# A convolution by Fourier steps with a token-wise network: one PSUM bank for the filter network's products, three PSUM buffers for the fold

## The chip, the cores and the metric

The kernel runs on one core of a Trainium2 chip. The metric is the device time of one execution in microseconds, from its first to its last instruction and what lies around them. Lower is better.

## The reference

`x` and `v` are (2, 12480, 128) in fp32. The first part multiplies them, convolves the product along the sequence with a learned filter, and multiplies by `x` again. The filter comes from a small two-layer network on position embeddings, and fades out along the sequence. The second part is a token-wise network with a rational activation.

```python
h_filt = (np.maximum(pos_emb @ w1, 0.0) @ w2) * np.exp(-0.01 * pos)[:, None]
u = x * v
Uf, Hf = np.fft.rfft(u, n=2 * S, axis=1), np.fft.rfft(h_filt, n=2 * S, axis=0)
y = np.fft.irfft(Uf * Hf[None, :, :], n=2 * S, axis=1)[:, :S, :]
out = moe(x * y)          # w_in (128, 2048), rational function, w_out (2048, 128)
```

## The kernel before

The transform is split in two steps, N = 192 x 120, so that it becomes matrix products. The kernel has three stages with a barrier between them: the first goes from `x`, `v` and the position embeddings to `bent` in DRAM, the second from `bent` to `back`, the third from `back` through the network to the output. Only the first stage is touched, and what follows is about it alone.

The sequence is seen as 104 rows of J = 120. A block is JB = 4 of these 120 columns, so there are 30 blocks. For a block, the engines do this:

- SP loads `x_s`, `v_s` and `pos_s` (`load`, lines 170 to 177) and stores the result in two halves (`store`, 179 to 186).
- The filter network: PE transposes the embeddings (`transposes`, L305) into `posT_p`; ACT copies them to `posT` (L223); PE multiplies by `w1` (`hidden`, L314) into `hid_p`; ACT applies the ReLU (L230); PE multiplies by `w2` (`filter_rows`, L321) into `filt_p`; DVE multiplies by the window (`filt`, L270), into the filter's columns of `uh`.
- DVE multiplies x and v (`product`, L264) into the other columns of `uh`.
- ACT rounds `uh` to `uh_hi` in two halves (`split_hi`, L239), and POOL subtracts to get `uh_lo` (`split_lo`, L211).
- For each of the four columns, PE folds (`fold_j`, L333): six matmuls of 384 columns into one buffer of `g_p` (two PSUM banks). ACT scales it by a cosine (`cos_part`, L246), DVE adds the sine part in two instructions (`turn`, L283 and L285) to `bent_s`. The second of these frees the buffer: `turned[j % 2]`.

PSUM holds eight banks. `posT_p`, `hid_p` and `filt_p` take one each, `g_p` has two buffers of two banks.

The order on each engine is written out by hand. `pipelined` (lines 86 to 102) runs a list of parts per step; a part with lead n works on the block n ahead. Step b on PE is: `transposes` of block b+2, fold 0 of b, `hidden` of b+2, fold 1 of b, `filter_rows` of b+2, fold 2 of b, fold 3 of b. On ACT: `posT` copy of b+2, cosine part 0 of b, `split_hi(0)` of b+1, ReLU of b+2, cosine part 1, `split_hi(1)` of b+1, cosine parts 2 and 3. On DVE: turn 0, `product` of b+2, turn 1, `filt` of b+2, turns 2 and 3. On SP: the store of b, then the load of b+5, which waits until the product of b+3 has been made. Each engine works through its list in that order; the semaphores between them carry counts of blocks or of folds. In the steady part a hardware loop covers two blocks per pass.

These waits matter for the change: `fold_j` waits for `turned[j % 2]` (L330), that is for the turn two folds before. `transposes` waits until the earlier copy has been taken out of `posT_p` (L302). `hidden` waits in addition for the earlier ReLU (L312), and `filter_rows` for the earlier `filt` (L319).

Of the kernel before, what the change touches and what calls it, by code (L numbers as in the profile page):

```python
# [38 lines left out]
JB = 4  # L39
# [5 lines left out]
SLOTS = 2  # L45
EPS = 1e-6
# [3 lines left out]
assert ROWS * J == SEQ and J_BLOCKS % SLOTS == 0 and K_BLOCKS % SLOTS == 0  # L50
# [22 lines left out]
def hyena_mlp(nc, x, v, pos_emb, w1, w2, w_in, w_out, a, b, tab, out):  # L73
# [30 lines left out]
    with ExitStack() as whole:  # L104
# [22 lines left out]
        with ExitStack() as ctx:  # L127
# [32 lines left out]
            g_done, part_done, turned = sem("g_done"), sem("part_done"), sems("turned")  # L160
# [3 lines left out]
            ITERS = J_BLOCKS // SLOTS  # L164
# [3 lines left out]
            @block.sync  # L168
            def _(sp):
                def load(i, s):  # L170
                    blk = i * SLOTS + s
# [7 lines left out]
                def store(i, s):  # L179
                    blk = i * SLOTS + s  # L180
# [10 lines left out]
                pipelined(sp, ITERS, SLOTS, [(0, store), (LEAD_LOAD, load)])  # L191
                for dst, src in ((spread_s, tab["spread"]), (turn_j, tab["turn_j"]), (unfold_s, tab["unfold"]), (w_in_s, w_in),
                                 (w_out_s, w_out.rearrange("(t p) d -> p t d", p=128)),
                                 (coef, a.rearrange("(o n) -> o n", o=1).to_broadcast([128, 4])),
                                 (den_raw, b.rearrange("(o n) -> o n", o=1).to_broadcast([128, 2]))):
                    sp.dma_start(dst[:], src).then_inc(later_in, 16)
                for out_sem in bent_out:
                    sp.wait_ge(out_sem, 16 * ITERS)

            @block.gpsimd  # L200
            def _(pool):

                for s in range(SLOTS):
                    nc.gpsimd.memset(uh[64:ROWS, s, :, BD:COLS], 0.0).then_inc(pad_zero, 1)

                def split_lo(i, s):
                    for half in range(2):

                        pool.wait_ge(uh_hi_done, (i * SLOTS + s) * 2 + half + 1)
# [4 lines left out]
                pipelined(pool, ITERS, SLOTS, [(0, split_lo)])  # L214

            @block.scalar
            def _(act):
                def posT_copy(i, s):
                    blk = i * SLOTS + s
# [3 lines left out]
                    nc.scalar.activation(posT[:], posT_p[:, 0:JB * FILTER_ROWS], ACT.Copy).then_inc(posT_sb, 1)  # L223

                def relu(i, s):
                    blk = i * SLOTS + s
# [3 lines left out]
                    nc.scalar.activation(hid[:], hid_p[:, 0:JB * FILTER_ROWS], ACT.Relu).then_inc(hid_sb, 1)  # L230

                def split_hi(half):
                    def part(i, s):
                        blk = i * SLOTS + s
# [7 lines left out]
                def cos_part(j):  # L242
                    def part(i, s):
                        n = (i * SLOTS + s) * JB + j
                        act.wait_ge(g_done, n + 1)
                        nc.scalar.activation(part_s[:, j % 2], g_p[0:K1, j % 2, :, 0:COLS], ACT.Copy,  # L246
# [6 lines left out]
                pipelined(act, ITERS, SLOTS, [(LEAD_MAKE, posT_copy), (0, cos_part(0)), (LEAD_SPLIT, split_hi(0)),  # L253
# [4 lines left out]
            def _(dve):  # L258
                def product(i, s):
                    blk = i * SLOTS + s  # L260
                    dve.wait_ge(xv_in[s], 32 * (i + 1))
# [5 lines left out]
                def filt(i, s):  # L267
                    blk = i * SLOTS + s
                    dve.wait_ge(filt_ps, blk + 1)
                    nc.vector.tensor_tensor(  # L270
                        uh[0:FILTER_ROWS, s, :, BD:COLS], filt_p[0:FILTER_ROWS],
# [3 lines left out]
                def turn(j):  # L275
                    def part(i, s):
                        n = (i * SLOTS + s) * JB + j
                        dve.wait_ge(part_done, n + 1)
                        if j % 2 == 0:
                            dve.wait_ge(bent_out[s * 2 + j // 2], 16 * i)  # L280
                        sin = turn_k[:, bass.ds(n, 1), 1:2].rearrange("p a b -> p (a b)")
                        neg = turn_k[:, bass.ds(n, 1), 2:3].rearrange("p a b -> p (a b)")
                        nc.vector.scalar_tensor_tensor(out=bent_s[:, s, j, 0, :], in0=g_p[0:K1, j % 2, 1, 0:COLS], scalar=sin,  # L283
                                                       in1=part_s[:, j % 2, 0, :], op0=ALU.mult, op1=ALU.add)
                        nc.vector.scalar_tensor_tensor(out=bent_s[:, s, j, 1, :], in0=g_p[0:K1, j % 2, 0, 0:COLS], scalar=neg,  # L285
                                                       in1=part_s[:, j % 2, 1, :], op0=ALU.mult, op1=ALU.add
                                                       ).then_inc(turned[j % 2], 1)
# [6 lines left out]
                pipelined(dve, ITERS, SLOTS, [(0, turn(0)), (LEAD_MAKE, product), (0, turn(1)), (LEAD_MAKE, filt),  # L294
# [3 lines left out]
            def _(pe):  # L298
                def transposes(i, s):
                    pe.wait_ge(pos_in[s], 16 * (i + 1))  # L300
                    if positive(i * SLOTS + s):
                        pe.wait_ge(posT_sb, i * SLOTS + s)  # L302
                    pe.sem_inc(pe_passed, 1)
                    for j in range(JB):
                        mm = nc.tensor.transpose(posT_p[:, j * FILTER_ROWS:(j + 1) * FILTER_ROWS], pos_s[:, s, j, :],  # L305
# [3 lines left out]
                def hidden(i, s):  # L309
# [4 lines left out]
                    nc.tensor.matmul(hid_p[:, 0:JB * FILTER_ROWS], w1_s[:], posT[:], start=True, stop=True).then_inc(hid_ps, 1)  # L314

                def filter_rows(i, s):
                    pe.wait_ge(hid_sb, i * SLOTS + s + 1)
                    if positive(i * SLOTS + s):
                        pe.wait_ge(filt_done, i * SLOTS + s)  # L319
                    for j in range(JB):  # L320
                        mm = nc.tensor.matmul(filt_p[0:FILTER_ROWS, j, :], hid[:, j * FILTER_ROWS:(j + 1) * FILTER_ROWS],  # L321
# [3 lines left out]
                def fold_j(j):  # L325
                    def part(i, s):
                        blk = i * SLOTS + s
                        if j % 2 == 0:
                            pe.wait_ge(uh_lo_done, blk * 2 + j // 2 + 1)
                        pe.wait_ge(turned[j % 2], blk * (JB // 2) + j // 2)  # L330
                        for c in range(2):
                            for n, (w, f) in enumerate(((fold_lo, uh_hi), (fold_hi, uh_hi), (fold_hi, uh_lo))):
                                mm = nc.tensor.matmul(g_p[0:K1, j % 2, c, 0:COLS], w[:, c * K1:(c + 1) * K1], f[:, s, j, :],  # L333
                                                      start=(n == 0), stop=(n == 2))
# [5 lines left out]
                pipelined(pe, ITERS, SLOTS, [(LEAD_MAKE, transposes), (0, fold_j(0)), (LEAD_MAKE, hidden), (0, fold_j(1)),  # L340
# [615 lines left out]
```

## Time and profile before

| what | value |
|---|---|
| median of three runs | 2239.24 us (2235.86 to 2241.52) |
| profiled execution | 2240.67 us |
| its span, first to last instruction | 2238.9 us |
| busy in the span: PE, DVE, ACT, POOL | 92%, 81%, 81%, 85% |
| first stage, by the timeline | to about 276 us |
| second stage | to about 640 us |
| third stage | the rest |

The busy shares are means over three stages that have little in common, so they say little about one of them. Times in the rows further down are microseconds from the start of the span. In a timeline row the first number is the start, the second the length, and the bracket tells how long the engine had been idle and what ended that; a row can merge several instructions of one kind ("x4"). A matmul's length includes its way through the array, so the next one starts before it ends.

### The profile page before, as it was taken

The numbers are of one execution on the slowest core, as the hardware profiler recorded it, in microseconds if no ns is written. First come the engines' busy times: TensorE is split into PE (matmuls) and PEld (weight loads), VectorE is DVE, ScalarE is ACT, GpSimd is POOL, SyncE is SP. The second block draws the span as 40 slices with busy tenths as digits, with TensorE's granted clock in tenths as the row PEclk, the third lists the DMA queues.
The fourth block names the chain that finished last, engine by engine and source line by source line (L and its number), as shares of the span: only waits on it lengthen the run. The fifth ranks groups of instructions, "written<-read, shape, count | busy, mean of one in ns | idle before, by whom it ended". The sixth has DMA issues, their size and how long they took to land. (4 is left out here: it accounts for less than half of the span.)

```text
span 2238.9 us, 33664 instructions
## 1 busy us (share of the span) xinstructions
PE 2048.9 (92%) x8964; PEld 1458.6 (65%) x8964; DVE 1805.7 (81%) x2271; ACT 1822.0 (81%) x2431; POOL 1894.0 (85%) x1218
## 2 busy tenths in 40 slices
PE   7888769999968999999999999999999999999997
PEld 5666559999955666666666666666666666666664
DVE  4777648888847888888888888888888888888887
ACT  4767646666638999999999999999999999899997
POOL 3666558888838999999999999999999999999997
PEclk9999979999979999999999999999999999999999
DMA  6888677666640111111111111111111111111100
GB/s 164 260 258 259 209 163 176 176 176 176 176 108 11 30 34 30 29 35 49 29 29 29 29 29 29 29 31 31 29 31 46 37 29 29 29 29 29 29 8 16
DMA packets 65724, 175.02 MB, mean 78 GB/s; under 512 B 5046, under 2 KB 8414, under 8 KB 62686
## 3 DMA queue, kind: packets, MB, share of 16 engines
q1 hardware_dynamic: 65694, 174.67, 29.4%
q8 instruction: 13, 0.21, 0.0%
q14 instruction: 17, 0.14, 0.0%
HBM read 102.89 MB, written 71.76 MB: 78 GB/s over the span
## 5 line engine op out<-in xcount | busy, mean ns | idle before, releaser
L625 POOL TENSOR_TENSOR den<-slope,mag 128x832 f32<-128x832 f32 x480 | 946.2, 1971 | 43.5 <-POOL slope L617 6.9
L878 PE MATMUL acc_p<-g_s,w_out_k 128*128 128x416 f32 x1920 | 784.1, 531 | 88.3 <-DVE g_s L785 83.5
L752 DVE SCALAR_TENSOR_TENSOR num<-square,level,h_p 128x832 f32<-128x832 f32 x480 | 517.8, 1079 | 90.1 <-ACT square L659 79.3
L617 POOL TENSOR_SCALAR slope<-mag,den_c 128x832 f32<-128x832 f32 x480 | 500.3, 1042 | 98.9 <-ACT mag L650 70.2
L785 DVE SCALAR_TENSOR_TENSOR g_s<-num,ratio,r_p 128x832 f32<-128x832 f32 x480 | 516.0, 1075 | 83.2 <-ACT r_p L676 54.6
L878 PEld LDWEIGHTS acc_p<-g_s,w_out_k 128*128 128x128 f32 x1920 | 332.6, 189 | 373.4 <-issue 221.8
L659 ACT ACTIVATE square<-h_p,centre 128x832 f32<-128x832 f32 x480 | 459.0, 956 | 128.7 <-DVE mag L747 112.5
L867 PE MATMUL h_p<-xy_hi,w_lo 128*128 128x416 f32 x960 | 459.1, 478 | 5.6 <-DVE num L752 4.3
L669 ACT ACTIVATE den<-den 128x832 f32<-128x832 f32 x480 | 431.1, 898 | 0.0
L676 ACT ACTIVATE r_p<-den 128x832 f32<-128x832 f32 x480 | 417.4, 870 | 12.9 <-DVE g_s L785 12.9
L867 PE MATMUL h_p<-xy_lo,w_hi 128*128 128x416 f32 x960 | 338.0, 352 | 0.0
L867 PE MATMUL h_p<-xy_hi,w_hi 128*128 128x416 f32 x960 | 337.5, 352 | 0.0
L867 PEld LDWEIGHTS h_p<-xy_hi,w_lo 128*128 128x128 f32 x960 | 181.6, 189 | 143.1 <-DVE num L752 113.0
L211 POOL TENSOR_TENSOR uh_lo<-uh,uh_hi 104x768 fp32r<-104x768 f32 x60 | 151.6, 2544 | 113.9 <-ACT uh_hi L239 113.8
L747 DVE TENSOR_SCALAR mag<-h_p 128x832 int32<-128x832 int32 x240 | 244.1, 1017 | 0.0
L409 POOL TENSOR_TENSOR bin_lo<-bin_s,bin_hi 120x768 fp32r<-120x768 f32 x96 | 178.3, 1858 | 71.2 <-ACT bin_hi L428 71.2
L867 PEld LDWEIGHTS h_p<-xy_hi,w_hi 128*128 128x128 f32 x960 | 182.4, 190 | 52.2 <-issue 51.4
L650 ACT ACTIVATE mag<-h_p 128x832 f32<-128x832 f32 x240 | 205.8, 857 | 3.2 <-PE h_p L867 3.2
L867 PEld LDWEIGHTS h_p<-xy_lo,w_hi 128*128 128x128 f32 x960 | 181.4, 189 | 1.4
L246 ACT ACTIVATE part_s<-g_p,turn_k 96x768 f32<-96x768 f32 x120 | 107.7, 898 | 83.0 <-PE g_p L333 83.0
L498 PE MATMUL x_p<-bin_hi,spread_lo 120*120 120x384 f32 x384 | 130.2, 339 | 28.5 <-POOL bin_lo L409 28.5
L498 PE MATMUL x_p<-bin_lo,spread_hi 120*120 120x384 f32 x384 | 130.6, 340 | 0.0
(79 smaller groups left out, 2805.4 us busy)
## 6 DMA issues: line engine op xcount, KB each, us to landing
bent<-bent_s SPq DMA_DIRECT2D x60, 576.0 KB, 4.8
bin_s<-bent SPq DMA_DIRECT2D x24, 1440.0 KB, 9.7
x_s<-in_x SPq DMA_DIRECT2D x60, 416.0 KB
back<-back_s SPq DMA_DIRECT2D x24, 960.0 KB, 7.8
vin_s<-back SPq DMA_DIRECT2D x30, 768.0 KB, 5.8
v_s<-in_v SPq DMA_DIRECT2D x30, 416.0 KB
out<-o_s SPq DMA_DIRECT2D x60, 208.0 KB
pos_s<-in_pos_emb SPq DMA_DIRECT2D x30, 88.0 KB
```

The costliest lines, as they stand in the source:

```text
L498: mm = nc.tensor.matmul(to, w, f, start=(n == 0), stop=(n == len(every) - 1))
L617: nc.gpsimd.tensor_scalar(slope[:, q % DEEP], mag[:, q % DEEP], den_c[:, 1:2], den_c[:, 0:1], ALU.mult, ALU.add).then_inc(slope_done, 1)
L625: nc.gpsimd.tensor_tensor(den[:, q % DEEP], slope[:, q % DEEP], mag[:, q % DEEP], ALU.mult).then_inc(den_done, 1)
L650: nc.scalar.activation(mag[:, q % DEEP], h_p[:, q % 2, :, 0:TOK], ACT.Abs).then_inc(mag_act, 1)
L659: nc.scalar.activation(square[:, q % SQUARES], h_p[:, q % 2, :, 0:TOK], ACT.Square, bias=centre[:]).then_inc(square_done, 1)
L669: nc.scalar.activation(den[:, q % DEEP], den[:, q % DEEP], ACT.Ln, bias=1.0 + EPS).then_inc(log_done, 1)
L676: nc.scalar.activation(r_p[:, :, 0:TOK], den[:, q % DEEP], ACT.Exp, scale=-1.0).then_inc(r_done, 1)
L747: nc.vector.tensor_scalar(mag[:, q % DEEP].bitcast(I32), h_p[:, q % 2, :, 0:TOK].bitcast(I32), NO_SIGN, None, ALU.bitwise_and).then_inc(ma ...
L752: nc.vector.scalar_tensor_tensor(out=num[:, q % NUMS], in0=square[:, q % SQUARES], scalar=level[:], in1=h_p[:, q % 2, :, 0:TOK], op0=ALU.a ...
L785: nc.vector.scalar_tensor_tensor(out=g_s[:, q % DEEP], in0=num[:, q % NUMS], scalar=ratio[:, 0:1], in1=r_p[:, :, 0:TOK], op0=ALU.add, op1= ...
L867: mm = nc.tensor.matmul(h_p[:, q % 2, t, 0:TOK], w[:, at:at + 128], f[:, s, b_, :], start=(n == 0), stop=(n == 2))
L878: mm = nc.tensor.matmul(acc_p[:, 0:TOK], w_out_k[:, ft], g_s[:, q % DEEP, t], start=(ft == 0), stop=(ft == FT - 1))
```

## The change

The three products of the filter network go to one bank, `mlp_p`, one after another. Two banks come free, and `g_p` gets a third buffer. Folds are numbered through, and fold n uses buffer n mod 3, so the loop is written over 6 blocks (24 folds) instead of 2; every count and slot is rewritten for that. The leads and the order of parts on each engine stay the same.

```diff
+RING = 3
...
-            part_s = sb("part_s", [K1, 2, 2, COLS])
+            part_s = sb("part_s", [K1, RING, 2, COLS])
...
-            posT_p = ps("posT_p", [ORDER, 512])
-            hid_p = ps("hid_p", [ORDER, 512])
-            filt_p = ps("filt_p", [128, JB, D])
-            g_p = ps("g_p", [128, 2, 2, 512])
+            mlp_p = ps("mlp_p", [128, 512])
+            g_p = ps("g_p", [128, RING, 2, 512])
...
-            ITERS = J_BLOCKS // SLOTS
+            PER = SLOTS * RING
+            ITERS = J_BLOCKS // PER
...
                     for half in range(2):
-                        sp.wait_ge(turned[1], blk * (JB // 2) + half + 1)
+                        last = q * JB + (half + 1) * (JB // 2) - 1
+                        sp.wait_ge(turned[last % RING], i * (PER * JB // RING) + last // RING + 1)
...
-                        nc.scalar.activation(part_s[:, j % 2], g_p[0:K1, j % 2, :, 0:COLS], ACT.Copy,
+                        r = (q * JB + j) % RING
+                        nc.scalar.activation(part_s[:, r], g_p[0:K1, r, :, 0:COLS], ACT.Copy,
...
-                                                       ).then_inc(turned[j % 2], 1)
+                                                       ).then_inc(turned[r], 1)
...
-                def transposes(i, s):
-                    pe.wait_ge(pos_in[s], 16 * (i + 1))
-                    if positive(i * SLOTS + s):
-                        pe.wait_ge(posT_sb, i * SLOTS + s)
+                def transposes(i, q):
+                    s = q % SLOTS
+                    pe.wait_ge(pos_in[s], 16 * (i * RING + q // SLOTS + 1))
+                    if positive(i * PER + q):
+                        pe.wait_ge(filt_done, i * PER + q)
...
-                    pe.wait_ge(posT_sb, i * SLOTS + s + 1)
-                    if positive(i * SLOTS + s):
-                        pe.wait_ge(hid_sb, i * SLOTS + s)
+                    pe.wait_ge(posT_sb, i * PER + q + 1)
...
-                    pe.wait_ge(hid_sb, i * SLOTS + s + 1)
-                    if positive(i * SLOTS + s):
-                        pe.wait_ge(filt_done, i * SLOTS + s)
+                    pe.wait_ge(hid_sb, i * PER + q + 1)
...
-                        pe.wait_ge(turned[j % 2], blk * (JB // 2) + j // 2)
+                        r = (q * JB + j) % RING
+                        pe.wait_ge(turned[r], i * (PER * JB // RING) + (q * JB + j) // RING)
```

## Rows read from the trace of the kernel before

**Rows 1.** Windows, warm stretch; busy us by engine, granted clock, DMA share, GB/s.
```profile
46.79:235.92 189.13, 163.64 (x874) 115.08 (x875) 142.59 (x230) 132.16 (x186) 118.52 (x46) 1.00 0.83 254
```

**Rows 2.** Waits from 40 to 230 us: waiter, releaser, total us, times, longest.
```profile
POOL uh_lo L211 <- ACT uh_hi L239: 77.6, 24, 7.0
...
PE g_p L333 <- DVE bent_s L285: 10.2, 23, 0.7
PE g_p L333 <- POOL uh_lo L211: 8.8, 11, 0.8
```

**Rows 3.** Timeline of one period: start us, length us, engine, line, idle before.
```profile
235.92 0.38 PE L333 MATMUL g_p<-uh_hi,fold_lo 104*96 104x384 f32 x1 [0.72 <-DVE bent_s L285]
...
237.32 0.90 ACT L246 ACTIVATE part_s<-g_p,turn_k 96x768 f32<-96x768 f32 x1 [1.04 <-PE g_p L333]
...
238.12 0.83 ACT L239 ACTIVATE uh_hi<-uh 104x768 fp32r<-104x768 f32 x1
...
238.38 0.61 DVE L283 SCALAR_TENSOR_TENSOR bent_s<-g_p,turn_k,part_s 96x384 f32<-96x384 f32 x1 [1.15 <-ACT part_s L246]
...
238.85 0.45 ACT L230 ACTIVATE hid<-hid_p 64x352 f32<-64x352 f32 x1
...
239.35 1.10 PE L321 MATMUL filt_p<-w_s,hid 64*88 64x128 f32 x8 [0.21 <-ACT hid L230]
239.43 1.21 DVE L264 TENSOR_TENSOR uh<-x_s,v_s 104x1024 f32<-104x1024 f32 x1
...
240.38 0.42 PE L333 MATMUL g_p<-uh_hi,fold_lo 104*96 104x384 f32 x1
...
240.57 0.61 DVE L283 SCALAR_TENSOR_TENSOR bent_s<-g_p,turn_k,part_s 96x384 f32<-96x384 f32 x1
...
241.62 0.68 DVE L270 TENSOR_TENSOR uh<-filt_p,window 88x512 f32<-88x512 f32 x1
...
241.75 0.41 PE L333 MATMUL g_p<-uh_hi,fold_lo 104*96 104x384 f32 x1
241.81 0.90 ACT L246 ACTIVATE part_s<-g_p,turn_k 96x768 f32<-96x768 f32 x1 [0.90 <-PE g_p L333]
...
242.87 0.47 PE L305 MATMUL posT_p<-ident,pos_s 88*64 88x88 f32 x4
242.87 0.61 DVE L283 SCALAR_TENSOR_TENSOR bent_s<-g_p,turn_k,part_s 96x384 f32<-96x384 f32 x1 [0.57 <-ACT part_s L246]
243.17 0.90 ACT L246 ACTIVATE part_s<-g_p,turn_k 96x768 f32<-96x768 f32 x1 [0.46 <-PE g_p L333]
...
243.97 0.44 ACT L223 ACTIVATE posT<-posT_p 64x352 f32<-64x352 f32 x1
...
244.16 0.38 PE L333 MATMUL g_p<-uh_hi,fold_lo 104*96 104x384 f32 x1 [0.82 <-POOL uh_lo L211]
```

**Rows 4.** Timeline, blocks 1 and 2: transposes and first folds on PE.
```profile
33.71 0.79 PE L305 MATMUL posT_p<-ident,pos_s 88*64 88x88 f32 x4
...
34.48 0.60 PE L333 MATMUL g_p<-uh_hi,fold_lo 104*96 104x384 f32 x1
...
46.79 0.39 PE L333 MATMUL g_p<-uh_hi,fold_lo 104*96 104x384 f32 x1 [0.36 <-DVE bent_s L285]
```

**Rows 5.** Timeline, start of the stage: second transposes and first filter product.
```profile
16.32 0.80 PE L305 MATMUL posT_p<-ident,pos_s 88*64 88x88 f32 x4
16.43 0.69 DVE L270 TENSOR_TENSOR uh<-filt_p,window 88x512 f32<-88x512 f32 x1 [4.83 <-PE filt_p L321]
```

**Rows 6.** Timeline, end of the stage: folds 0 of blocks 28, 29; last turn.
```profile
260.61 0.38 PE L333 MATMUL g_p<-uh_hi,fold_lo 104*96 104x384 f32 x1 [1.12 <-POOL uh_lo L211]
...
267.63 0.38 PE L333 MATMUL g_p<-uh_hi,fold_lo 104*96 104x384 f32 x1 [0.80 <-DVE bent_s L285]
...
275.22 0.60 DVE L285 SCALAR_TENSOR_TENSOR bent_s<-g_p,turn_k,part_s 96x384 f32<-96x384 f32 x1
```

**Rows 7.** Windows, stretch behind the stage, columns as in rows 1.
```profile
278.00:305.30 27.30, 4.07 (x13) 4.07 (x14) 2.73 (x2) 3.88 (x4) 3.58 (x2) 0.50 0.89 208
```

More of the change, by code:

```diff
@@ L48 @@
 NO_SIGN = 0x7FFFFFFF
-assert ROWS * J == SEQ and J_BLOCKS % SLOTS == 0 and K_BLOCKS % SLOTS == 0
+assert ROWS * J == SEQ and J_BLOCKS % (SLOTS * RING) == 0 and K_BLOCKS % SLOTS == 0
 assert N >= SEQ + FILTER_ROWS * J - 1 and FILTER_ROWS <= ROWS <= 128 and TOK <= 512
@@ L169, in _, with load @@
             def _(sp):
-                def load(i, s):
-                    blk = i * SLOTS + s
+                def load(i, q):
+                    blk, s = i * PER + q, q % SLOTS
                     if positive(blk - 1):
@@ L190, in _ @@
                     sp.dma_start(dst[:], src).then_inc(consts_in, 16)
-                pipelined(sp, ITERS, SLOTS, [(0, store), (LEAD_LOAD, load)])
+                pipelined(sp, ITERS, PER, [(0, store), (LEAD_LOAD, load)])
                 for dst, src in ((spread_s, tab["spread"]), (turn_j, tab["turn_j"]), (unfold_s, tab["unfold"]), (w_in_s, w_in),
@@ L197, in _ @@
                 for out_sem in bent_out:
[L198 removed]
+                    sp.wait_ge(out_sem, 16 * (J_BLOCKS // SLOTS))
             @block.gpsimd
@@ L204, in _, with split_lo @@
                     nc.gpsimd.memset(uh[64:ROWS, s, :, BD:COLS], 0.0).then_inc(pad_zero, 1)
-                def split_lo(i, s):
+                def split_lo(i, q):
+                    s = q % SLOTS
                     for half in range(2):
-                        pool.wait_ge(uh_hi_done, (i * SLOTS + s) * 2 + half + 1)
+                        pool.wait_ge(uh_hi_done, (i * PER + q) * 2 + half + 1)
                         at = slice(half * (JB // 2), (half + 1) * (JB // 2))
@@ L212, in split_lo, with posT_copy @@
                                                 ALU.subtract).then_inc(uh_lo_done, 1)
-                pipelined(pool, ITERS, SLOTS, [(0, split_lo)])
+                pipelined(pool, ITERS, PER, [(0, split_lo)])
             @block.scalar
             def _(act):
-                def posT_copy(i, s):
-                    blk = i * SLOTS + s
+                def posT_copy(i, q):
+                    s = q % SLOTS
+                    blk = i * PER + q
                     act.wait_ge(posT_ps, blk + 1)
@@ L222, in posT_copy, with relu @@
                         act.wait_ge(hid_ps, blk)
-                    nc.scalar.activation(posT[:], posT_p[:, 0:JB * FILTER_ROWS], ACT.Copy).then_inc(posT_sb, 1)
-                def relu(i, s):
-                    blk = i * SLOTS + s
+                    nc.scalar.activation(posT[:], mlp_p[0:ORDER, 0:JB * FILTER_ROWS], ACT.Copy).then_inc(posT_sb, 1)
+                def relu(i, q):
+                    s = q % SLOTS
+                    blk = i * PER + q
                     act.wait_ge(hid_ps, blk + 1)
@@ L229, in relu, with part @@
                         act.wait_ge(filt_ps, blk)
-                    nc.scalar.activation(hid[:], hid_p[:, 0:JB * FILTER_ROWS], ACT.Relu).then_inc(hid_sb, 1)
+                    nc.scalar.activation(hid[:], mlp_p[0:ORDER, 0:JB * FILTER_ROWS], ACT.Relu).then_inc(hid_sb, 1)
                 def split_hi(half):
-                    def part(i, s):
-                        blk = i * SLOTS + s
+                    def part(i, q):
+                        s = q % SLOTS
+                        blk = i * PER + q
                         act.wait_ge(filt_done, blk + 1)
@@ L252, in _ @@
                 nc.scalar.activation(fold_hi[:], fold[:], ACT.Copy).then_inc(split_done, 1)
-                pipelined(act, ITERS, SLOTS, [(LEAD_MAKE, posT_copy), (0, cos_part(0)), (LEAD_SPLIT, split_hi(0)),
+                pipelined(act, ITERS, PER, [(LEAD_MAKE, posT_copy), (0, cos_part(0)), (LEAD_SPLIT, split_hi(0)),
                                               (LEAD_MAKE, relu), (0, cos_part(1)), (LEAD_SPLIT, split_hi(1)),
@@ L258, in _, with product @@
             def _(dve):
-                def product(i, s):
-                    blk = i * SLOTS + s
-                    dve.wait_ge(xv_in[s], 32 * (i + 1))
+                def product(i, q):
+                    s = q % SLOTS
+                    blk = i * PER + q
+                    dve.wait_ge(xv_in[s], 32 * (i * RING + q // SLOTS + 1))
                     if positive(blk - 1):
@@ L293, in _ @@
                 nc.vector.tensor_tensor(fold_lo[:], fold[:], fold_hi[:].bitcast(F32), ALU.subtract).then_inc(split_done, 1)
-                pipelined(dve, ITERS, SLOTS, [(0, turn(0)), (LEAD_MAKE, product), (0, turn(1)), (LEAD_MAKE, filt),
+                pipelined(dve, ITERS, PER, [(0, turn(0)), (LEAD_MAKE, product), (0, turn(1)), (LEAD_MAKE, filt),
                                               (0, turn(2)), (0, turn(3))])
@@ L298, in _, with hidden, filter_rows @@
             def _(pe):
-                def transposes(i, s):
-                    pe.wait_ge(pos_in[s], 16 * (i + 1))
-                    if positive(i * SLOTS + s):
-                        pe.wait_ge(posT_sb, i * SLOTS + s)
+                def transposes(i, q):
+                    s = q % SLOTS
+                    pe.wait_ge(pos_in[s], 16 * (i * RING + q // SLOTS + 1))
+                    if positive(i * PER + q):
+                        pe.wait_ge(filt_done, i * PER + q)
                     pe.sem_inc(pe_passed, 1)
                     for j in range(JB):
-                        mm = nc.tensor.transpose(posT_p[:, j * FILTER_ROWS:(j + 1) * FILTER_ROWS], pos_s[:, s, j, :],
+                        mm = nc.tensor.transpose(mlp_p[0:ORDER, j * FILTER_ROWS:(j + 1) * FILTER_ROWS], pos_s[:, s, j, :],
                                                  ident[0:FILTER_ROWS, 0:FILTER_ROWS])
                     mm.then_inc(posT_ps, 1)
-                def hidden(i, s):
-                    pe.wait_ge(posT_sb, i * SLOTS + s + 1)
-                    if positive(i * SLOTS + s):
-                        pe.wait_ge(hid_sb, i * SLOTS + s)
+                def hidden(i, q):
+                    s = q % SLOTS
+                    pe.wait_ge(posT_sb, i * PER + q + 1)
                     pe.sem_inc(pe_passed, 1)
-                    nc.tensor.matmul(hid_p[:, 0:JB * FILTER_ROWS], w1_s[:], posT[:], start=True, stop=True).then_inc(hid_ps, 1)
-                def filter_rows(i, s):
-                    pe.wait_ge(hid_sb, i * SLOTS + s + 1)
-                    if positive(i * SLOTS + s):
-                        pe.wait_ge(filt_done, i * SLOTS + s)
+                    nc.tensor.matmul(mlp_p[0:ORDER, 0:JB * FILTER_ROWS], w1_s[:], posT[:], start=True, stop=True).then_inc(hid_ps, 1)
+                def filter_rows(i, q):
+                    s = q % SLOTS
+                    pe.wait_ge(hid_sb, i * PER + q + 1)
                     for j in range(JB):
-                        mm = nc.tensor.matmul(filt_p[0:FILTER_ROWS, j, :], hid[:, j * FILTER_ROWS:(j + 1) * FILTER_ROWS],
+                        mm = nc.tensor.matmul(mlp_p[0:FILTER_ROWS, j * D:(j + 1) * D], hid[:, j * FILTER_ROWS:(j + 1) * FILTER_ROWS],
                                               w2_s[:], start=True, stop=True)
@@ L325, in fold_j, with part @@
                 def fold_j(j):
-                    def part(i, s):
-                        blk = i * SLOTS + s
+                    def part(i, q):
+                        s = q % SLOTS
+                        blk = i * PER + q
                         if j % 2 == 0:
                             pe.wait_ge(uh_lo_done, blk * 2 + j // 2 + 1)
-                        pe.wait_ge(turned[j % 2], blk * (JB // 2) + j // 2)
+                        r = (q * JB + j) % RING
+                        pe.wait_ge(turned[r], i * (PER * JB // RING) + (q * JB + j) // RING)
                         for c in range(2):
-                            for n, (w, f) in enumerate(((fold_lo, uh_hi), (fold_hi, uh_hi), (fold_hi, uh_lo))):
-                                mm = nc.tensor.matmul(g_p[0:K1, j % 2, c, 0:COLS], w[:, c * K1:(c + 1) * K1], f[:, s, j, :],
-                                                      start=(n == 0), stop=(n == 2))
+                            for term, (w, f) in enumerate(((fold_lo, uh_hi), (fold_hi, uh_hi), (fold_hi, uh_lo))):
+                                mm = nc.tensor.matmul(g_p[0:K1, r, c, 0:COLS], w[:, c * K1:(c + 1) * K1], f[:, s, j, :],
+                                                      start=(term == 0), stop=(term == 2))
                         mm.then_inc(g_done, 1)
@@ L339, in _ @@
                 pe.wait_ge(split_done, 2)
-                pipelined(pe, ITERS, SLOTS, [(LEAD_MAKE, transposes), (0, fold_j(0)), (LEAD_MAKE, hidden), (0, fold_j(1)),
+                pipelined(pe, ITERS, PER, [(LEAD_MAKE, transposes), (0, fold_j(0)), (LEAD_MAKE, hidden), (0, fold_j(1)),
                                              (LEAD_MAKE, filter_rows), (0, fold_j(2)), (0, fold_j(3))])
```

33 lines of the change are left out of this document (18 added, 15 removed).

## The prediction

> **What bounds the kernel now.** The change lies in the first stage alone, so I read the stage by itself: its windows first, then who waits for whom in it, then one period instruction by instruction. From the fold of block 2 on, no engine is full: in 189 us PE is busy 164 (its busy time counts the pipelined tail of each matmul), DVE 143, ACT 132, POOL 119, and the DMA engines are at 0.83 [rows 1]. What is to be seen: everything is partly idle, so a chain that closes on itself sets the period, and no engine's work does. The waits say where PE stands: it waits for DVE's turn (L285), and in nearly as many microseconds for POOL's `uh_lo` [rows 2]. The second I take to be wrongly named: the first half of `uh_lo`, which `fold_j(0)` needs, is ready long before, and only the end of the second half falls beside the end of the turn. POOL itself stands idle for 77.6 us waiting for ACT, so it isn't what is late.
>
> The period is read from fold 0 at 235.92 to the next fold 0 at 244.16, 8.24 us [rows 3]. Follow back what each start waited for. Fold 0 waits for turn 2 of the block before, because there are two PSUM buffers; turn 2 for the cosine part 2; that for fold 2; fold 2 stands on PE behind `filter_rows`; that waits for the ReLU; the ReLU stands on ACT behind `split_hi(0)`, that behind cosine part 0, and that waits for fold 0. In steps, from the starts in [rows 3]: fold 0 to cos 0 1.40, to split 0.80, to ReLU 0.73, to filter_rows 0.50, to fold 2 1.03, to cos 2 1.43, to turn 2 1.06, to the next fold 0 1.29. Sum 8.24: the whole period is explained. Fold 0 of block 2 starts at 46.79 and of block 28 at 260.61 [rows 4, 6], 26 periods of 8.22.
>
> Before 46 us the same chain does not bind. Fold 0 of blocks 1 and 2 start at 34.48 and 46.79, 12.31 apart, and the same matmul takes 0.60 there and 0.39 afterwards [rows 4]: the array is at the lower of its two levels, 1.2 GHz, and PE's own queue fills the period. (The clock column has no entry for the time before its first change; the matmul's length tells.)
>
> **The change, part by part.**
>
> Third PSUM buffer, removed wait: fold n waits for turn n-3 instead of n-2. Fold 0 of the next block then needs turn 1 of this one. Taking fold 0 as time 0, turn 1 starts at 4.65 [rows 3], so with the 1.29 of above it frees the buffer at 5.94. The last three links (1.43 + 1.06 + 1.29 = 3.78) leave the chain.
>
> What is late next: PE's own order. Fold 2 starts 4.46 after fold 0, as before, since cos 0, split, ReLU and filter_rows are not touched. Behind it come fold 3, the transposes for two blocks ahead, and the next fold 0. A fold takes PE 1.12 until the next thing can start (fold 3 to transposes, 241.75 to 242.87 [rows 3]). Fold 3 now needs only turn 0, which starts at 2.46 and frees its buffer before 3.75: no wait. So fold 3 at 5.58, transposes at 6.70. From transposes to fold 0 without a wait the warm trace has nothing; at the low clock it is 0.77 (33.71 to 34.48 [rows 4]). Half of that, 0.39, is the lower bound, all of it the upper; I take 0.50, near the lower, because four small matmuls scale with the clock and only the issue gap doesn't. New period 4.46 + 1.12 + 1.12 + 0.50 = **7.20**, against 8.22: 1.02 saved per block.
>
> One bank for three products, added wait: the transposes now wait for `filt_done` of the block before; until now they waited only for the copy out of their own bank (`posT_sb`). Queued behind them on PE is fold 0, and behind it everything. `filt` starts at 5.70 and takes 0.68 [rows 3], so with 0.1 for the semaphore the wait ends at 6.48, and PE reaches it at 6.70: 0.22 of slack, cost nothing. What hides it is fold 3. If that cover goes, each tenth costs 26 x 0.1 = 2.6 us. The waits dropped in `hidden` and `filter_rows` were met already: nothing.
>
> The start of the stage has no such cover. The second transposes start at 16.32, while the first `filt` starts at 16.43 and takes 0.69 [rows 5]: they would wait until 17.2, 0.9 later. The third transposes stand the same way to the second `filt`, and fold 0 of block 0 stands behind them. Cost 2 x 0.9 = 1.8 us; bounds 0 (if the first operands are late anyway) and 2.5. Against this the 0.36 that fold 0 of block 2 waits for DVE goes [rows 4].
>
> The loop over 6 blocks instead of 2, the shared semaphores counted by thirds, and SP's `store` waiting for the third's own semaphore: SP waits for the same turns as before, 1 and 3. No DMA is added or moved on SP's or POOL's queue. Cost 0; bounds: a loop jump saved or a longer body fetched, less than 1 us either way from how exactly 26 periods agree with the sum of one.
>
> Other queues at 7.20: ACT would start cos 3 at 5.58 + 1.42 = 7.00 and copy `posT` at 7.80 (0.80 after it, as at 243.17 and 243.97 [rows 3]), done at 8.24, before cos 0 of the next block is due at 8.60. DVE would begin the next turn 0 at 9.66 and is done with turn 3 by 9.3. DMA: 0.83 x 8.22 = 6.8 us of transfers per block, 0.95 of a period of 7.20. Loads are issued five blocks ahead, so a queue that is nearly full delays nothing yet.
>
> End of the stage: fold 0 of blocks 28 and 29 start 7.02 apart and the last turn starts 7.59 after the second [rows 6]. With three buffers and no filter work the chain for block 28 is fold 0, cos 0 and split (2.20), cos 1 (0.73 more), turn 1 (1.06), release (1.29): 5.2, saving 1.8. In block 29 fold 3 waits for turn 0 (2.46 + 1.29 = 3.75) where it now waits for turn 1; to the last turn 3.8 + 1.42 + 1.06 + 0.53 = 6.8, saving 0.8. The last full period has no transposes behind it, 0.5 more.
>
> **Sum:** 26 x 1.02 = 26.5; + 0.5 + 1.8 + 0.8 = 29.6; - 1.8 at the start, + 0.36: **28.2 us**. The stages behind begin after a barrier and are not changed; they shift as a whole. The profiled execution took 2240.67 and would take 2212.5; it lies 1.4 above the median of the three runs, so from the median 2239.24 - 28.2 = **2211.0**.
>
> **Rivals.**
>
> A, *DMA becomes the bound.* For: 0.95 of the period needed. Against: the same engines reach 0.89 over a 27 us stretch with other work [rows 7], and the transfers of a block are queued in time. If 0.90 is the most they give here, the period is 6.82/0.90 = 7.58, the gain 26 x 0.64 + 1.3 = 18, the time 2221. Chance 0.14.
>
> B, *the new wait takes the old one's place*, or the third buffer is never used. DVE must bring `filt` before 6.70; if `filt` came 1.24 later than in [rows 3], the period would be what it was and the time within 6 us of 2239. For: only 0.22 of slack, and product and turn 1 stand ahead of `filt` on DVE. Against: its chain from fold 0 (1.40 + 1.06 + 1.05 + 1.14 + 1.05 to `filt`) has no step that the change makes longer. Chance 0.08. The Trainium skill (TensorE: Matmul & The Clock Gate, HAM oscillation) tells of a matmul kernel where more PSUM buffering gave no further gain. By that the sum would be 0; here the trace speaks against it, since PE's named wait in this stage is for exactly that buffer [rows 2].
>
> C, *slower: the array falls to 1.2 GHz inside the stage.* PE now waits on one bank between copy and product, and cycles through three buffers. A block at the low clock costs 12.31 instead of 7.20 [rows 4], 5.1 more. From 6 such blocks on (28.2/5.1) the gain is gone; with half of the 26 low it is 2211 + 13 x 5.1 = 2277. The trace shows such a fall when PE had stopped at the end of the stage: the clock is 0.50 from 278.0 to 305.3 with PE busy for 4.07 [rows 7]. Against: with waits in every block the clock stays 1.00 through 189 us [rows 1], and the change makes PE denser. Chance 0.07. The Trainium skill speaks for C (the same page, A second HAM failure mode: psum-queue depth-cycling): cycling through PSUM banks leaves small idle gaps between groups of matmuls, and the clock then swings. By that rule the kernel before should swing as well, and rows 1 show that it doesn't.
>
> D, *the clock rises earlier.* Blocks 0 and 1 run at 12.3. If the rise falls ahead of them both, 2 x 5.1 = 10 us more are saved: 2201. Chance 0.05. A rise later by 3 us costs about 1.
>
> **The numbers.** Forecast 0.66, A 0.14, B 0.08, C 0.07, D 0.05. The forecast's own bounds: transposes to fold 0 between 0.39 and 0.77 gives 26 x (-0.11 to +0.27) = -2.9 to +7; runs lie 5.7 apart (2235.86 to 2241.52), so 3 either way. That makes 2205 to 2220; with A and part of D **2202 to 2224**. About 0.3% (6.7 us) is what a measurement can tell from no change. Faster 0.85 (forecast, A, D), same 0.08 (B), slower 0.07 (C).
>
> **What would show it.** In the profile after: fold 0 to fold 0 about 7.2; PE's wait for L285 nearly gone and no wait for `filt` (L270) past the first blocks; fold 3 right behind fold 2; DMA share about 0.95 in the same stretch; fold 0 of block 0 later by 1.8; clock 1.00 from about 46 us to the stage's end. Wrong if the period is above 7.6 (then see whether DVE waits for a load, or PE for `filt`), or if the clock shows 0.50 inside the stage.

## The result and the profile after

The changed kernel takes 2198.32 us in the median of 4 runs (2197.26 to 2199.37), against 2237.78 for the kernel before (4 runs, 2235.86 to 2241.52). The ratio is 0.982, with a 95% interval of 0.9806 to 0.9834: 39.5 us less, where 28.2 were forecast. The direction was right; the size was 11 us short and the time lies below the forecast range. In later comparisons, with more runs of the kernel before, its median was 2240.3 to 2241.5, so the gain is rather 41 to 43 us. In the two profiled executions the spans are 2238.9 and 2195.5, 43.4 apart.

The window of the warm stretch of the kernel after, as [rows 1] (columns: stretch, its length, busy us of PE, weight loads, DVE, ACT and POOL, granted clock, DMA share, GB/s):

```profile
44.22:216.14 171.92, 167.76 (x951) 125.88 (x950) 152.91 (x251) 143.89 (x201) 129.09 (x51) 1.00 0.93 308
```

PE is now busy for 168 of 172 us, and the DMA engines for 0.93 instead of 0.83. In the waits of that stretch (40 to 200 us), both lines of [rows 2] in which PE waits at the fold, for DVE's turn and by name for POOL, are absent, and so is any wait of PE for `filt`:

```profile
POOL uh_lo L213 <- ACT uh_hi L244: 45.2, 24, 6.0
ACT part_s L253 <- PE g_p L345: 20.6, 47, 0.9
DVE bent_s L294 <- ACT part_s L253: 17.7, 45, 0.6
...
PEld mlp_p L331 <- ACT hid L234: 8.5, 24, 0.6
PE mlp_p L325 <- ACT posT L226: 3.9, 23, 0.2
```

One period on the timeline, the counterpart of [rows 3] (L345 is the fold, L253 the cosine part, L244 the rounding, L234 the ReLU, L331 `filter_rows`, L325 `hidden`, L317 the transposes, L226 the copy of `posT`, L279 `filt`):

```profile
188.09 0.40 PE L345 MATMUL g_p<-uh_hi,fold_lo 104*96 104x384 f32 x1
...
188.94 0.44 ACT L226 ACTIVATE posT<-mlp_p 64x352 f32<-64x352 f32 x1
...
189.49 0.90 ACT L253 ACTIVATE part_s<-g_p,turn_k 96x768 f32<-96x768 f32 x1
...
189.53 0.77 PE L325 MATMUL mlp_p<-posT,w_s 64*64 64x352 f32 x2 [0.17 <-ACT posT L226]
...
190.23 0.42 PE L345 MATMUL g_p<-uh_hi,fold_lo 104*96 104x384 f32 x1
190.29 0.83 ACT L244 ACTIVATE uh_hi<-uh 104x768 fp32r<-104x768 f32 x1
...
191.03 0.45 ACT L234 ACTIVATE hid<-mlp_p 64x352 f32<-64x352 f32 x1
...
191.52 1.10 PE L331 MATMUL mlp_p<-w_s,hid 64*88 64x128 f32 x8
...
192.56 0.41 PE L345 MATMUL g_p<-uh_hi,fold_lo 104*96 104x384 f32 x1
...
193.68 0.33 PE L345 MATMUL g_p<-uh_hi,fold_lo 104*96 104x384 f32 x1
...
193.80 0.68 DVE L279 TENSOR_TENSOR uh<-mlp_p,window 88x512 f32<-88x512 f32 x1
...
193.98 1.94 ACT L253 ACTIVATE part_s<-g_p,turn_k 96x768 f32<-96x768 f32 x2 [0.69 <-PE g_p L345]
...
194.72 0.47 PE L317 MATMUL mlp_p<-ident,pos_s 88*64 88x88 f32 x4
...
194.97 0.40 PE L345 MATMUL g_p<-uh_hi,fold_lo 104*96 104x384 f32 x1
```

Fold 0 to fold 0 is 188.09 to 194.97, **6.88 us** (8.24 before, 7.20 forecast). The start of the stage, as [rows 4] and [rows 5]:

```profile
22.88 0.69 DVE L279 TENSOR_TENSOR uh<-mlp_p,window 88x512 f32<-88x512 f32 x1 [4.37 <-PE mlp_p L331]
...
23.71 0.77 PE L317 MATMUL mlp_p<-ident,pos_s 88*64 88x88 f32 x4 [0.87 <-DVE uh L279]
...
35.76 0.79 PE L317 MATMUL mlp_p<-ident,pos_s 88*64 88x88 f32 x4
...
36.26 0.61 PE L345 MATMUL g_p<-uh_hi,fold_lo 104*96 104x384 f32 x1
...
43.12 0.47 PE L317 MATMUL mlp_p<-ident,pos_s 88*64 88x88 f32 x4
...
43.38 0.40 PE L345 MATMUL g_p<-uh_hi,fold_lo 104*96 104x384 f32 x1
```

The transposes of step 0 (23.71) wait for `filt`, by name. Fold 0 of block 1 starts at 36.26, where it was 34.48: 1.78 later. In parts: the first transposes start 0.26 later (11.29 against 11.03, both waiting for the first load), from there to fold 0 of block 0 it takes 1.79 more (12.91 against 11.12), which is the wait for `filt`, and block 0 takes 0.27 less (12.06 against 12.33). But fold 0 of block 2 starts at 43.38, where it was 46.79: block 1 took 7.12 instead of 12.31. The first matmul of fold 0 is 0.61 long in block 1 and 0.40 in block 2, so the array's rise from 1.2 to 2.4 GHz lies between them; the clock record of this execution has it at 36.8 us, that of the kernel before at 45.9. (All rises below are the first change in the clock record, on the scale of the timeline; the expectations call this one 36.5.) And the end of the stage, as [rows 6]: fold 0 of block 28, and the last instruction of the last turn.

```profile
221.93 0.34 PE L345 MATMUL g_p<-uh_hi,fold_lo 104*96 104x384 f32 x1
...
233.29 0.60 DVE L296 SCALAR_TENSOR_TENSOR bent_s<-g_p,turn_k,part_s 96x384 f32<-96x384 f32 x1
```

**Where the 43.4 us came from**, and what had been forecast for each:

| part | before | after | gain | forecast |
|---|---|---|---|---|
| to fold 0 of block 1 | 34.48 | 36.26 | -1.8 | -1.8 |
| to fold 0 of block 2 | 12.31 | 7.12 | +5.2 | +0.4 |
| 26 periods, to fold 0 of block 28 | 213.8 | 178.6 | +35.3 | +27.0 |
| to the last turn | 14.6 | 11.4 | +3.3 | +2.6 |
| everything behind | 1963.7 | 1962.2 | +1.5 | 0 |

The last line is no gain. Over the profiles of all kernels here it lies between 1961.8 and 1965.7, without order. So two terms were off: the period by 8.3 us, and the block in which the clock rises by 4.8.

### The profile page after: what moved, and what is told of

Same layout as the page of the kernel before. It is cut to its first block and busy times, and to the rows that moved or that the text cites. A ratio compares the mean times of both kernels' runs of the same rounds, so it can differ in the third digit from the quotient of the medians.

```text
span 2195.5 us, 33367 instructions
## 1 busy us (share of the span) xinstructions
PE 2032.1 (93%) x8964; PEld 1456.4 (66%) x8964; DVE 1803.5 (82%) x2271; ACT 1822.5 (83%) x2431; POOL 1894.3 (86%) x1218
## 5 line engine op out<-in xcount | busy, mean ns | idle before, releaser
L253 ACT ACTIVATE part_s<-g_p,turn_k 96x768 f32<-96x768 f32 x120 | 107.7, 898 | 38.6 <-PE g_p L345 31.9
L858 PE MATMUL m_p<-vin_s,unfold 96*104 96x512 f32 x240 | 116.6, 609 | 15.1 <-DMA vin_s<-back 13.9
```

## The experiments

Two theories stood at the outset. The first: the third buffer makes all of the gain, the shared bank costs 2 us at the start, and the chain of the forecast is right but for the sizes. Its rival: something else has a part, the longer loop body, POOL's `uh_lo`, the transfers, or the clock. Periods below are means between the copies of `posT` for blocks 5 and 27 (22 periods, in one profile of each kernel); by that measure the kernel before has 8.222 and the changed one 6.883.

**E1, shared bank with two buffers, loop over 6.** `GB` is 2; the slots of `part_s` and the counts of `turned` go by `GB` too (not shown).

```diff
-            g_p = ps("g_p", [128, RING, 2, 512])
+            g_p = ps("g_p", [128, GB, 2, 512])
```

> The changed kernel with two fold buffers instead of three: the shared bank and the loop over 6 blocks stay. Theory (all of the gain is the third buffer's, the shared bank costs only at the start): period 8.2 us as before, start later by about 2, total within 3 us of the kernel before, 2236 to 2241. Rival (the longer loop body or the shared bank brings part of the gain): period under 8.0, total under 2232. If the earlier rise of the clock (36.5 instead of 45.9 us) comes from the third buffer, it stays late here.

Measured: 2238.85 (10 runs, 2236.03 to 2245.21), ratio 0.9994 [0.9979, 1.0008]. Period 8.143. The third buffer is what matters: without it there is no gain. The clock rose at 35.6 us in this profile, so an early rise doesn't need the third buffer. The period is 0.08 shorter than before, which asked for E4.

**E2, filter rows in a bank of their own, three buffers.** The transposed embeddings and the hidden layer still share one, and the total is eight banks. The second edit below is in `transposes`; `filter_rows` waits for `filt_done` again (not shown).

```diff
+            filt_p = ps("filt_p", [128, 512])
...
-                        pe.wait_ge(filt_done, i * PER + q)
+                        pe.wait_ge(hid_sb, i * PER + q)
```

> The changed kernel, but only the transposed embeddings and the hidden layer share a bank; the filter rows get a bank of their own, and the fold keeps three buffers. The transposes wait for the ReLU before them instead of for the window product. Theory: period 6.89 as in the changed kernel, the start of the stage earlier by 1.8, total 2196.5. Rival (the wait for the window product costs in every block too): period under 6.8, total under 2193.

Measured: 2197.36 (2195.75 to 2199.18), beside 2199.30 for the changed kernel in the same comparison (2196.62 to 2201.44). Period 6.895. The copy of `posT` in step 0 starts at 22.27 instead of 24.55, 2.28 earlier. But 0.50 of that is the first load, which landed earlier in this execution (the first copy is at 11.55 against 12.05); from first copy to third it is 10.72 against 12.50. So the wait for `filt` costs 1.8 us once, and nothing per block. The medians are 1.9 apart, with runs that overlap.

**E3, the kernel before with the ReLU ahead of the first rounding.**

```diff
-                pipelined(act, ITERS, SLOTS, [(LEAD_MAKE, posT_copy), (0, cos_part(0)), (LEAD_SPLIT, split_hi(0)),
-                                              (LEAD_MAKE, relu), (0, cos_part(1)), (LEAD_SPLIT, split_hi(1)),
+                pipelined(act, ITERS, SLOTS, [(LEAD_MAKE, posT_copy), (0, cos_part(0)), (LEAD_MAKE, relu),
+                                              (LEAD_SPLIT, split_hi(0)), (0, cos_part(1)), (LEAD_SPLIT, split_hi(1)),
```

> The kernel before, with one edit: ACT does the ReLU ahead of the first half of the rounding, which takes 0.73 us out of the chain. Theory (the chain over ReLU, filter_rows, fold 2, turn 2 sets the period): the period falls from 8.22 to about 7.6, where DVE's order of turns takes over, total about 2222. Rival (PE waits for POOL's uh_lo, as its wait of 8.8 us says): POOL starts 0.43 later, the period stays or grows, total 2238 or more.

Measured: 2234.43 (10 runs, 2229.11 to 2240.30), ratio 0.998 [0.9963, 0.9997], period 7.933. The chain is real, since the period fell, and POOL is not it: it began 3.45 after fold 0 instead of 3.11, the period fell all the same, and no wait of PE is named after it in 50 to 220 us. But of 0.62 expected only 0.29 came, and the total fell by 7 in the medians where 2222 had been expected. The timeline of this kernel shows why (L314 `hidden`, L246 cosine part 0, L333 fold 1, L230 ReLU, L321 `filter_rows`):

```profile
202.79 0.80 PE L314 MATMUL hid_p<-posT,w_s 64*64 64x352 f32 x2
202.99 0.90 ACT L246 ACTIVATE part_s<-g_p,turn_k 96x768 f32<-96x768 f32 x1 [0.82 <-PE g_p L333]
...
203.52 0.42 PE L333 MATMUL g_p<-uh_hi,fold_lo 104*96 104x384 f32 x1
...
203.79 0.45 ACT L230 ACTIVATE hid<-hid_p 64x352 f32<-64x352 f32 x1
...
204.74 1.10 PE L321 MATMUL filt_p<-w_s,hid 64*88 64x128 f32 x8
```

The ReLU ends at 204.24, and `filter_rows` still starts only at 204.74: fold 1 holds PE from 203.52 on. The path over PE's own queue (fold 0, `hidden`, fold 1, `filter_rows`) lies 0.3 behind the path over ACT, and the forecast had not listed it.

The ten times fall into three groups: 2229.1 to 2229.3, 2233.9 to 2234.7 and 2238.9 to 2240.3. The steps are near what one more block at the low clock costs (12.3 against 7.9). That fits a rise of the clock that comes later in some executions; only one of the ten has a profile, 2229.11 with the rise at 34.7.

**The changed kernel again**, without an edit.

> The changed kernel once more. Same total, 2198. If the time at which the clock rises is an accident of the execution, it lies elsewhere than at 36.5 us in this profile; if it follows from the program, it is there again.

Measured: 2199.30 (2196.62 to 2201.44), period 6.883, rise at 35.5 us. The early rise is not tied to one instant, but stays near it.

**E4, the shared bank alone in the loop over 2.** The kernel before with `mlp_p` for the three products and the transposes waiting for `filt_done`.

> The kernel before with the shared bank alone: two fold buffers, loop over 2 blocks. In the experiment with the loop over 6 blocks the period was 8.14 instead of 8.22. If the loop's length made those 0.08, the period here is 8.22; if the shared bank did, 8.14. Start of the stage 2 us later than before either way. Where does the clock rise: near 35 us as in four of five profiles so far, or near 46.

Measured: one run, 2246.83; period 8.200. So the shared bank leaves the period nearly alone (0.02), and the loop over 6 blocks brings 0.06 of the 0.08: some 1.5 us in all, from one profile of each. The clock rose at 60.4, later than in any other profile. Its transposes and first folds of blocks 2 and 3 (L303 and L327; lengths tell the level):

```profile
47.79 0.79 PE L303 MATMUL mlp_p<-ident,pos_s 88*64 88x88 f32 x4
...
48.56 0.60 PE L327 MATMUL g_p<-uh_hi,fold_lo 104*96 104x384 f32 x1
...
60.11 0.60 PE L303 MATMUL mlp_p<-ident,pos_s 88*64 88x88 f32 x4
...
60.87 0.39 PE L327 MATMUL g_p<-uh_hi,fold_lo 104*96 104x384 f32 x1 [0.16 <-DVE bent_s L283]
```

**E5, the changed kernel with the ReLU ahead** (the edit of E3).

> The changed kernel with the ReLU ahead of the first half of the rounding on ACT. Theory A (chain over ReLU and filter_rows as forecast, next bound DVE's order): the period falls from 6.88 to about 6.74. Theory B (a second closed chain stands right behind it: cosine part 3, posT copy, hidden, fold 1, filter_rows, fold 2, fold 3, cosine part 3 = 0.81 + 0.59 + 0.70 + 1.22 + 1.04 + 1.12 + 1.34 = 6.82): the period falls to 6.82 only.

Measured: one run, 2198.71, period 6.840. This is near theory B's 6.82 and not A's 6.74: with three buffers a second closed chain runs about 0.05 behind the first.

**E6, a new order.** On the layout of E2, with the ReLU ahead. The orders are given here in words, not as the code has them:

```text
-  PE:  transposes(b+2), fold 0, hidden, fold 1, filter_rows, fold 2, fold 3
+  PE:  fold 0, hidden, fold 1, filter_rows, fold 2, transposes(b+3), fold 3
-  ACT: posT_copy(b+2), cos 0, split 0, relu, cos 1, split 1, cos 2, cos 3
+  ACT: cos 0, relu, split 0, cos 1, split 1, cos 2, posT_copy(b+3), cos 3
```

> Three fold buffers, filter rows in their own bank, and a new order: the transposes of block b+3 stand between fold 2 and fold 3, their copy between cosine parts 2 and 3, the ReLU ahead of the first rounding. Theory B: hidden no longer waits for the copy, and PE's own queue sets the period: 1.19 + 0.73 + 1.12 + 1.04 + 1.12 + 0.25 + 1.04 = 6.5, total about 2188. Rival (the DMA engines, at 0.93 of 6.89 = 6.4, cannot be used above 0.93): period stays at 6.8 or more, total 2196 or more.

Measured: 2198.59 (2197.61 to 2202.42), period 6.906. A miss. Single periods are 6.6, near the forecast, but others are 6.9 to 7.5 and one is 7.8, and the waits of 60 to 200 us name a cause that neither side had: the transposes one block further ahead need `pos_s` earlier than it lands.

```profile
PE mlp_p L318 <- DMA pos_s<-in_pos_emb: 3.8, 9, 1.0
```

Over these 140 us that is 0.19 per block, about what separates 6.91 from the 6.73 of E10. E6 has a second loss at the end of the stage, shown under E10.

**E7, PE kept busy at the start.** The changed kernel with matmuls whose result nobody uses: 26 before the first transposes, and 3 behind each of the first two transposes and the first two products of `hidden`:

```diff
+                def keep_busy(n):
+                    for _ in range(n):
+                        nc.tensor.matmul(g_p[0:K1, 0, 0, 0:2 * K1], fold_lo[:, 0:K1], fold_lo[:], start=True, stop=True)
...
+                    if isinstance(i, int) and i * PER + q < LEAD_MAKE:
+                        keep_busy(3)
...
                 pe.wait_ge(split_done, 2)
+                keep_busy(26)
```

> The changed kernel with matmuls added whose result nobody uses: 26 before the first transposes, 3 behind each of the first transposes and hidden products, so that PE is busy from 7 us on. Theory (the array rises to 2.4 GHz by what PE does, and late because it is sparse until 24 us): the matmuls are at the higher level before the first fold, block 0 takes 7 instead of 12.3 us, total 5 to 9 us less, 2190 to 2194, and the runs agree better with each other. Rival (the time of the rise does not hang on PE's work): it lies at 35 us, total 2199 or more.

Measured: 2196.86 (2196.72 to 2199.57), rise at 35.9. A miss: though PE worked from 6.7 us on, with pauses of up to 0.9, the rise stayed where it was.

**E8, the kernel before with PE's pause filled.** The pause is the 0.27 us for which PE waits for the turn between transposes and fold 0 at the low clock (0.77 against 0.50). `spare_p` is a bank that was free.

```diff
                     mm.then_inc(posT_ps, 1)
+                    for _ in range(2):
+                        nc.tensor.matmul(spare_p[0:K1, 0:2 * K1], fold_lo[:, 0:K1], fold_lo[:], start=True, stop=True)
```

> The kernel before (two fold buffers) with two matmuls of 192 columns behind each transposes, into a spare bank, read by nobody. They fill the 0.27 us in which PE waits for the turn in a block at the low clock, as the third buffer does, and lie inside that wait at the high clock. Theory (PE's short waits before 46 us are what let the clock rise late in some executions): all executions rise near 35 us, the times lie within 5 us of each other near 2235, none at 2240 to 2247. Rival (the time of the rise is an accident): the times spread over 11 us as those of the kernel before, median 2240.

Measured: 2237.54, and all 12 runs within 2235.85 to 2238.99. The kernel before, in the same comparison, spread over 17 runs from 2236.47 to 2246.18, median 2240.98. Ratio 0.9985 [0.9976, 0.9993]. The period is 8.216, unchanged, and the profile has the rise at 34.8. Its timeline (L306 transposes, L310 the added matmuls, L336 fold; the wait for the turn is filled at the low clock, and hidden at the high one):

```profile
33.97 0.79 PE L306 MATMUL posT_p<-ident,pos_s 88*64 88x88 f32 x4
...
34.48 0.54 PE L310 MATMUL spare_p<-fold_lo 104*96 104x192 f32 x2
...
34.85 0.34 PE L336 MATMUL g_p<-uh_hi,fold_lo 104*96 104x384 f32 x1
...
42.00 0.39 PE L310 MATMUL spare_p<-fold_lo 104*96 104x192 f32 x2
```

Added work made the kernel faster in the median. None of the 12 runs is above 2239.0, where 13 of the 17 of the kernel before are above 2240, so what it took away are most likely the executions with a late rise; one profile of E8, with an early rise, is all that shows the clock itself. The third buffer takes away the same 0.27 (block 0 takes 12.06 instead of 12.33), and no profile with it has a late rise. That it acts on the clock in this way is the reading that fits both, and is not shown apart.

**E9, the changed kernel without the loads of x from block 2 on.** It uses the old x again, so its result is not the convolution.

> The changed kernel with the loads of x left out from block 2 on (the old x is used again), a fifth of the stage's bytes. Theory (the chain of engines sets the period of 6.88, the DMA engines at 0.93 only follow): period 6.88, total within 3 us of 2198. Rival (the DMA engines hold the period): period down to 6.7 or less, total under 2194.

Measured: one run, 2196.32, period 6.879. The window from 60 to 200 us:

```profile
60.00:200.00 140.00, 136.53 (x776) 102.72 (x776) 124.71 (x205) 116.82 (x163) 106.03 (x41) 1.00 0.81 247
```

A DMA share of 0.81 instead of 0.93, and the same period (6.883 before the edit): the transfers don't hold it.

**E10, the copy ahead of cosine part 3.** PE's order as in the changed kernel, E2's banks, on ACT: cos 0, relu, split 0, cos 1, split 1, cos 2, posT_copy(b+3), cos 3.

> Three fold buffers and filter rows in their own bank; PE's order as in the changed kernel; on ACT the ReLU ahead of the first rounding, and the copy of the next step's transposes ahead of cosine part 3. Theory (both closed chains over ACT cut, PE's own queue left: 1.20 + 0.73 + 1.12 + 1.04 + 1.12 + 1.04 + 0.26): period 6.5 to 6.6, total about 2188. Rival (6.41 us of transfers cannot be fitted in 6.55): period 6.75 to 6.9, total 2194 to 2198.

**E11, the same without the loads of x.**

> The kernel of the experiment before this one with the loads of x left out from block 2 on. If its period is that of the full loads, the engines' chain sets it; if it is shorter, the transfers do. PE's queue gives 6.5.

Measured for E10: 2197.00 (2195.61 to 2200.85), ratio 0.9807 [0.9791, 0.9823], period 6.730; for E11 one run, 2196.82, period 6.698. Windows from 60 to 200 us, E10 and then E11:

```profile
60.00:200.00 140.00, 138.76 (x787) 104.40 (x786) 127.46 (x208) 118.28 (x167) 101.33 (x43) 1.00 0.92 311
```

```profile
60.00:200.00 140.00, 139.24 (x790) 105.37 (x789) 128.27 (x210) 118.42 (x168) 102.08 (x42) 1.00 0.83 251
```

The period lies 0.15 below that of the changed kernel, between the two expectations, and the total is where the rival had it. But the rival's cause isn't it: with a DMA share of 0.83 instead of 0.92 the period moves by 0.03. PE is busy for 138.8 of 140 us: its own queue is now nearly all of the period, at 6.7 instead of the 6.5 summed from its single steps. The total is as good as E2's, and 1 to 2 us under the changed kernel's; intervals this wide don't rank them.

Why the shorter period doesn't show in the total stands behind the 22 periods. From fold 0 of block 24 to that of block 28 E10 takes 30.1 us, the changed kernel and E2 27.0, and this loss of 3.1 is nearly all that 0.15 per block had gained. In these blocks DVE's product (L273), started beside POOL's `uh_lo`, takes 2.6 to 2.8 instead of 1.21:

```profile
185.62 1.21 DVE L273 TENSOR_TENSOR uh<-x_s,v_s 104x1024 f32<-104x1024 f32 x1
...
207.16 2.78 DVE L273 TENSOR_TENSOR uh<-x_s,v_s 104x1024 f32<-104x1024 f32 x1
```

E6 and E11 show the same (29.9 and 30.1), so the loads of x are not its cause. What is stays open; no run was made for it.

## Why the prediction was right and where it was wrong

**Right.** The chain that bounded the kernel before, and its cut: E1 has the shared bank and no gain; with the third buffer the wait for the turn is gone. PE's wait named after POOL was a wrong name (E3). The wait for `filt` costs nothing per block and 1.8 us at the start, as forecast: 1.79 between the traces of before and after, 1.78 by E2. Rival A falls with E9: the engines give 0.93, and a fifth of the bytes less changes nothing. Rival B: the period didn't stay. Rival C: the granted clock is 1.00 from the rise to PE's last fold of the stage in every profile with three buffers. The rule of the Trainium skill behind C (TensorE: Matmul & The Clock Gate, A second HAM failure mode: psum-queue depth-cycling) is not borne out here: with three buffers instead of two PE is denser (168 busy of 172 us, before 164 of 189), and the clock doesn't swing. Nor does the Trainium skill's case in which more PSUM buffering gave nothing (the same page, HAM oscillation) carry over: PE's wait for a buffer was on the chain here, and with the third one 26 periods are 35 us shorter.

**Wrong, the period.** The step that failed is "from transposes to fold 0 ... 0.77 (33.71 to 34.48)", with half of it as the lower bound. That row was not free of the wait that the change removes. In the kernel before, the turn's second instruction of that block runs beside it:

```profile
33.72 0.61 DVE L285 SCALAR_TENSOR_TENSOR bent_s<-g_p,turn_k,part_s 96x384 f32<-96x384 f32 x1
```

It ends at 34.33, and fold 0 starts at 34.48, 0.15 later. In [rows 3], where the wait is long enough to be marked (0.82, there by the wrong name), the same instruction ends at 244.01 and fold 0 starts at 244.16, 0.15 later as well:

```profile
243.41 0.60 DVE L285 SCALAR_TENSOR_TENSOR bent_s<-g_p,turn_k,part_s 96x384 f32<-96x384 f32 x1
```

So the 0.77 holds the wait for the turn; the row gives it no name. Free of it, the changed kernel has 0.50 at the low clock (35.76 to 36.26) and 0.25 at the high one (194.72 to 194.97); the forecast had taken 0.50 for the high one. The other links came as forecast: 1.40, 0.80, 0.74, 0.49, 1.04, 1.12, then fold 3 in 1.04 instead of 1.12: right behind fold 2, its second matmul starts 0.17 after its first, where in fold 2, behind `filter_rows`, it is 0.25. The 0.25 and the 0.08 make the 0.32 by which 7.20 is too long; times 26 it is 8.3 us. The loop over 6 blocks, costed at nothing, may hold 1.5 of them (E1 against E4). The copy of `posT`, listed as done in time, was in truth level: `hidden` waits for it (0.17 in each of 23 blocks of the waits above), and it is what E5 ran into.

**Wrong, the clock.** The forecast left the rise where one profile had it, at 45.9, and gave 0.05 to rival D. Nine profiles of kernels with three buffers have it at 33.3 to 38.7. The four with two buffers and no filling have it at 34.7, 35.6, 45.9 and 60.4. The profile of before was one of the later ones, and so part of the 4.8 us is luck of that profile; the spread of 5.7 us over three runs was read as noise and is likely this. D holds for half of what it said: block 1 is fast, block 0 is not. E8 puts the share of the clock at 3.4 us in the medians (2240.98 to 2237.54). With the parts of the table that don't hang on the rise (35.3 + 3.3 - 1.8 = 36.8) that makes 40, beside 39.5 to 43 in the medians.

Open: what within PE's work before 45 us the rise hangs on. Filling the pause between transposes and fold 0 narrowed the times, filling the stretch before 24 us did nothing, and no run separates the other pauses of a block.

## What to carry to other kernels

When a wait is removed, what comes next is sized from rows that don't hold the same wait: lay the supposed releaser's end beside every "free" interval, since short waits have no name. Of a kernel bounded by a chain, write down the second chain too; here it lay 0.05 to 0.3 us behind and decided what every further edit brought. A few microseconds of spread between runs of one kernel can be a clock that rises at different times, and it is worth looking at several profiles before costing a block at the low clock. A period measured in the middle of a loop says nothing of its last blocks: E10 gained in one and lost it in the other.

## What the runs showed of the hardware

Two idle matmuls per block made a kernel faster (E8, ratio 0.9985 [0.9976, 0.9993]), although they are never used and the period at the high clock is the same. PE had paused 0.27 us in a block of 12.3 at the low level, and with such pauses the rise to 2.4 GHz came as late as 45.9 and 60.4 us in two profiles, and at 34.7 and 35.6 in two others; without the pause it came at 33.3 to 38.7 in ten. Work of PE before 24 us, 26 matmuls back to back from 6.7 us on, left it at 35.9 (E7). The DMA engines ran at a share of 0.93 and 308 GB/s over 172 us while no engine waited for them by name, where 0.90 had been the rival's ceiling. One and the same product on DVE (104 x 1024, fp32) took 1.21 us through most of the stage and 2.78 in its last blocks (E10).
